# Expert programs of one engine: a fixed place for the second half of each program's code, and one branch hint fewer

## The reference

```python
logits = x @ w_gate
expert_idx = np.argmax(logits, axis=1)
...
h = np.maximum(np.einsum('ecd,edf->ecf', disp, w1), 0.0)
y = np.einsum('ecf,efd->ecd', h, w2)
...
out[i] = gate_w[i] * y[expert_idx[i], pos[i]]
```

## Time and profile before

| what | value |
|---|---|
| median of 3 runs | 406.74 us (404.05 to 407.35) |
| time of the profiled execution | 404.03 us |
| its span, first to last instruction | 402.3 us |
| PE busy | 390.4 us, 97% |
| granted clock of TensorE | 0.999 |
| experts, from the first program's jump to the end | from about 266 to 402 us |

### The profile page before, as it was taken

How to read it: one execution, slowest core, us unless ns; L and a number is a source line. 1 busy time by engine, 2 the same in 40 slices (tenths; PEclk the granted TensorE clock), 3 DMA queues, 4 the chain that set the end, 5 groups by cost and what they waited for, 6 DMA issues and landing times.

```text
span 402.3 us, 7811 instructions
## 1 busy us (share of the span) xinstructions
PE 390.4 (97%) x2876; PEld 372.0 (92%) x2876; DVE 247.9 (62%) x546; ACT 212.4 (53%) x453; POOL 181.5 (45%) x172
## 2 busy tenths in 40 slices
PE   8999999999999999999999999989999999899996
PEld 4999989899999999999999999578999998899995
DVE  5976766745457755457755664658764475786422
ACT  3727766437435236435243333239865577886432
POOL 3865514510304030201039900264896578987542
PEclk9999999999999999999999999999999999999999
DMA  8999968221504051000046140177778787685010
GB/s 216 371 359 338 370 195 297 51 99 51 152 0 150 2 149 51 0 2 2 0 119 219 40 119 2 65 173 232 200 230 224 205 241 240 212 265 148 0 52 21
DMA packets 22716, 58.96 MB, mean 147 GB/s; under 512 B 3332, under 2 KB 8134, under 8 KB 22412
## 3 DMA queue, kind: packets, MB, share of 16 engines
q1 hardware_dynamic: 19052, 50.99, 40.7%
q0 software_dynamic: 2304, 5.77, 5.4%
q10 hardware_dynamic: 1312, 1.52, 1.1%
HBM read 52.46 MB, written 7.91 MB: 150 GB/s over the span
## 4 chain that ended last, share of the span: by engine, by line
PE 91%; DVE 3%; DMA 2%; issue 1%; ACT 1%; POOL 1%; POOLq 0%; SPq 0%; ACTq 0%
PE bank L1410 22%; PE bank L1418 11%; PE bank L1392 10%; PE bank L1393 9%; PE bank L1394 9%; PE bank L1297 5%; PE bank L1396 5%; PE bank L1395 5%; PE bank L1250 3%; PE bank L1280 2%; PE bank L1338 2%; PE bank L1266 2%; PE bank L1535 2%; DMA w2r<-in_w 1%; DMA xg<-xd,idg 1%
## 5 line engine op out<-in xcount | busy, mean ns | idle before, releaser
L798 ACT ACTIVATE tt<-bank 128x384 f32<-128x384 f32 x64 | 31.3, 489 | 76.7 <-PE bank L1396 74.6
L1135 DVE TENSOR_TENSOR g<-bank,tt 128x384 f32<-128x384 f32 x64 | 35.6, 557 | 46.6 <-ACT tt L798 46.3
L1151 DVE TENSOR_TENSOR gl<-g,gh 128x384 fp32r<-128x384 f32 x64 | 41.7, 652 | 29.1 <-ACT gh L808 29.0
L1410 PE MATMUL bank<-woh,gh 128*128 128x328 f32 (+1 forms) x189 | 59.1, 322 | 0.2 <-ACT gh L808 0.2
L1410 PE MATMUL bank<-wol,gh 128*128 128x328 f32 (+1 forms) x189 | 57.2, 311 | 0.0
L1167 DVE SCALAR_TENSOR_TENSOR gl<-bank,gh 128x384 fp32r<-128x384 f32 x64 | 35.4, 555 | 32.2 <-ACT gh L827 31.9
L560 POOL TENSOR_TENSOR w2l<-w2r,w2h 128x640 fp32r<-128x640 f32 x28 | 44.1, 1576 | 23.8 <-DVE w1l L896 23.5
L808 ACT ACTIVATE gh<-g 128x384 fp32r<-128x384 f32 x64 | 33.5, 523 | 37.0 <-DVE g L1135 37.0
L827 ACT ACTIVATE gh<-bank 128x384 fp32r<-128x384 f32 x64 | 31.4, 491 | 30.0 <-PE bank L1396 29.2
L551 POOL TENSOR_TENSOR y<-hs,eo 128x320 f32<-128x320 f32 x11 | 9.0, 815 | 82.1 <-DVE hs L961 71.2
L1392 PE MATMUL bank<-xh,wih 128*128 128x384 f32 x124 | 44.3, 357 | 0.0
(11 more groups left out here) (239 smaller groups left out, 1000.8 us busy)
## 6 DMA issues: line engine op xcount, KB each, us to landing
w1r<-in_w SPq DMA_DIRECT2D x32, 384.0 KB, 3.7
w2r<-in_w SPq DMA_DIRECT2D x32, 320.0 KB, 4.6
qkt<-in_qk SPq DMA_DIRECT2D x12, 416.0 KB
ee<-gsc SPq DMA_DIRECT2D x9, 512.0 KB, 8.8
nat<-in_nat SPq DMA_DIRECT2D x12, 372.0 KB, 7.9
wir<-in_w_in SPq DMA_DIRECT2D x4, 768.0 KB, 12.8
wt<-in_w_out_turned SPq DMA_DIRECT2D x2, 1536.0 KB, 15.9
wor<-in_w_out SPq DMA_DIRECT2D x4, 656.0 KB, 14.1
```

Source lines behind the costliest of these rows:

```text
L1135: ve.tensor_tensor(g[m % 2][:], ps_h[m % 2][:, 0:TM], tt[m % 2][:], ALU.max).then_inc(s_g, 1)
L1151: ve.tensor_tensor(gl[m % 3][:], g[m % 2][:], gh[m % 3][:].bitcast(F32), ALU.subtract)\
L1410: last = mm(parts[s], gh[m % 3][:, cols], w[:, f, 0:parts[s].shape[1]], start=f == 0 and i == 0, stop=False, skip_group_check=True)
```

## The change

```diff
+            BLOCK_AT = {1: (6, 86), 2: (FE, 108), 3: (FE, 88)}
...
             def arm(e, nt, nt_next):
-                near = pe.mark_branch_hint_location()
...
-                return near
...
                             if f == 4 and e + 1 < E:
                                 hints = announce(held[e + 1])
+                            if f == BLOCK_AT[nt][0] and e + 1 < E:
+                                pe.addr_align(256, offset=BLOCK_AT[nt][1], max_nops=0)
                             h_step(M2 + e * FE + f, nt)
...
                         if e + 1 < E:
+                            if FE == BLOCK_AT[nt][0]:
+                                pe.addr_align(256, offset=BLOCK_AT[nt][1], max_nops=0)
                             with pe.If_lt(held[e + 1], one):
-                                near = arm(e, nt, 1)
-                                pe.br(program(e + 1, 1)).branch_hint(hints[0]).branch_hint(near)
+                                arm(e, nt, 1)
+                                pe.br(program(e + 1, 1)).branch_hint(hints[0])
```

More of the change, by code:

```diff
@@ L1767, in _ @@
                         if e + 1 < E:
+                            if FE == BLOCK_AT[nt][0]:
+                                pe.addr_align(256, offset=BLOCK_AT[nt][1], max_nops=0)
                             with pe.If_lt(held[e + 1], one):
-                                near = arm(e, nt, 1)
-                                pe.br(program(e + 1, 1)).branch_hint(hints[0]).branch_hint(near)
+                                arm(e, nt, 1)
+                                pe.br(program(e + 1, 1)).branch_hint(hints[0])
                             with pe.Else():
                                 with pe.If_lt(held[e + 1], few):
-                                    near = arm(e, nt, 2)
-                                    pe.br(program(e + 1, 2)).branch_hint(hints[1]).branch_hint(near)
+                                    arm(e, nt, 2)
+                                    pe.br(program(e + 1, 2)).branch_hint(hints[1])
                                 with pe.Else():
-                                    near = arm(e, nt, 3)
-                                    pe.br(program(e + 1, 3)).branch_hint(hints[2]).branch_hint(near)
+                                    arm(e, nt, 3)
+                                    pe.br(program(e + 1, 3)).branch_hint(hints[2])
                         else:
```

## The result

The changed kernel takes 407.04 us, the median of 16 runs (405.59 to 413.34). The kernel before, run beside it, takes 404.29 us, also the median of 16 (402.82 to 408.98). The ratio is 1.0067 with a 95% interval of 1.0042 to 1.0093: about 2.7 us slower, where 2.2 us faster were forecast. The profiled execution of the changed kernel took 407.11 us.

What follows compares the result with a forecast made beforehand. PE's own work bounds the kernel (busy 97% of the span). -2.8 (experts 3, 4) + 0.3 (expert 5) + 0.3 (padding branches) = -2.2 us, from the 406.74 us median to 404.5 us; range 401.0 to 408.5.

Steps and rivals of the forecast that it cites:

- Gain, two misses: Far branches ending experts 3 and 4 (3.25 and 3.07 us) would find their target fetched in time: 2.80 us gained.
- Experts 0, 1, 2 and 6 lose nothing visible on PE now, so there is nothing to gain there: Far branches ending these four experts: no PE time lost before the change, so no gain counted, 0 us.
- its target's packet cannot be asked for sooner than now: Expert 5's jump from nt 1 to nt 3 stays late: 0.63 us loss remains and grows by 0.3 us (0 to 0.7).
- The branches over the padding: One added branch in each of seven programs, mostly covered by PE's queue: +0.3 us, between 0 and 1.1.
- What is next late: With PE 3 us earlier, the weight pieces on DVE and POOL come next but are not met: no cost.
- Median: The whole kernel's median was 2.7 us above the profiled execution; this unexplained difference was carried over, giving 404.5 us.
- Rival (a): Longer runs before had one or two more far-branch misses; a fixed layout recovers those too: 401.8 us, chance 0.20.
- (b): At the far branches the near hint, not the far hint, brought the target; five more miss: +6.7 us, 413.4 us, chance 0.12.
- (c): Fetch starts late behind the new block's entry; expert 3 stays missed, expert 4 at best late: 406 to 407.3 us, chance 0.15.

Runs made afterwards that it cites:

- mix: Changed kernel with new slots for nt 1 programs alone (40, for expert 6 61), so only their arms lie in one block: 407.43 us, ratio 1.0001.
- arms-in-block kernel: Changed kernel with slots 40, 50, 14 (expert 6: 61, 71, 14), all arms and far branches in the entered block: 405.60 us, ratio 0.9929; again 0.9956.

## Why the prediction was wrong

**Gain, two misses: right.** Forecast 1.25 + 1.55 us; the stages of experts 3 and 4 fell by 1.21 and 1.52, on branches of 0.66 and 0.39 us.

**"Experts 0, 1, 2 and 6 lose nothing visible on PE now, so there is nothing to gain there": this step failed.** I read it as "nothing changes" and put 0 for expert 1, which lost 2.50 us. I had the fact before me: the branch to `nt` 3 lies 40 to 67 slots into "the block behind it". I counted that only for the far branch's target. The block behind is itself code, and it too has to be brought in: its packet began at 294.3 us, and PE stood for 1.49 us. In a program with `nt` 2, as expert 1's, it is needed right after the entry, because the comparisons jump over the arms for `nt` 1 and 2 and land 14 slots ahead of it. Four runs carry this: the arms moved into one block bring expert 1 back to 16.38 and, again, to 16.42 us; the entry moved two steps earlier with the border left where it was, to 16.35; the mix leaves it at 18.91.

**Expert 5, "its target's packet cannot be asked for sooner than now", +0.3 us (0 to 0.7): the same failure.** Measured +2.32 us. That this step's direction was right helps little: I priced the 14 slots by how long the sequencer takes to issue them, 0.7 us, and not by how long it waits for blocks. Its entry lies two steps ahead of the arms, so the stop at the border held PE up by only 0.15 us, but the target's packet came at 364.1 us, 2.1 us behind that stop, where it came at 361.4 before. The quoted sentence holds for this layout alone: with the arms in one block the branch took 0.40 us. How large the loss is differs from one profile to another: stage 5 took 16.35, 15.58 (near hints kept) and 15.01 us (run again), against 14.03 before. Together the two experts cost 4.8 us where 0.3 was set down, and that alone turns the forecast of -2.2 into about +2.3.

**The branches over the padding, +0.3 us (0 to 1.1): close to 0.** They took 0.20 to 0.39 us each on the sequencer, more than the 0.2 assumed:

```profile
L1761 PEldq COMPARE_BRANCH  x3: 317/333/389, 275.7 to 357.1; - x3
L1772 PEldq COMPARE_BRANCH  x4: 201/262/322, 291.7 to 381.2; - x4
```

PE's queue covered them all: stages 0, 2, 4, 6 and 7 show no new cost, and no gap stands behind them at step 6. The feared place was one border too early. The last sentence of the prediction had a stall at the padding branch "if the block that it enters had not been fetched"; that block was there, and the one behind it was not. With these 0 us the sum is +2.1 us, as the stages say.

**What is next late: partly wrong.** It was DVE's xeh at expert 5 (PE waited 0.31 us), seen once the branch there took 0.40 us.

**Median: the carry-over failed by itself.** The 2.7 us between the profiled execution and the median of three was scatter: over 16 runs the kernel before has 404.29 us, 0.3 above the profiled one. With the sum alone, -2.2 on 404.3, I would have forecast 402.1. That the measured 407.04 us lies inside the stated 401.0 to 408.5 is luck, two errors that went against each other. Rival (a) rested on that same scatter and fell.

**Rivals (b) and (c).** (b) fell with the far hint alone (0.9992). That the far hints bring their targets is shown for the six long jumps, which take 0.39 to 0.47 us with hints (arms in one block) and 3.3 to 3.9 us without. It is not shown for the seventh, expert 6's: its target is in the next block in sequence, and it takes 0.30 us with a hint and 0.29 without. So the 0.33 us branch of the earlier trace rows, which is this one, says nothing for the hints; the 0.41 us branch does. (c) gave 406 to 407.3 us and its number was hit by luck: it counted from 406.74 us, a change of -0.7 to +0.6, and +2.7 was measured. Its course was missed too: it wanted expert 3 still missed, and expert 3 was cured. Its mechanism, a fetch that starts late behind an entry, is real at another place. In the changed kernel the first instruction packet lies 1.6 to 3.2 us behind the entry at experts 0, 1, 3, 4 and 5, and in the arms-in-block kernel 0.8 to 1.9 us at all seven. The longest, 3.2 us, is expert 0's, which lost nothing; at experts 1 and 5 it is 2.3 and 2.1 us. What decides there is not an unusually late packet but a second block that is needed behind the first.

## What to carry to other kernels

Where code is laid out by hand, count every block that the sequencer enters between the hint and the jump's target, and not only the block of the target: in these runs each came with a packet of its own, and where a branch or PE waited for it, went on 2.3 to 2.7 us behind the packet's start. Put the comparisons and all arms with their branches into one block that is entered ahead of them (two steps ahead in the `nt` 1 programs here, where one step left a gap of 0.32 us at expert 5); a jump over arms that landed 14 slots short of a border cost most here, 2.50 us. The same goes for the start of a program that is reached by an unannounced jump: five or six slots short of a border, it made PE wait 2.4 to 4.3 us more. And a branch that costs PE nothing today is no proof that its surroundings may be moved: ask what the new layout adds there too.

## What the runs showed that I had not expected

- The near hint shows no effect, within 0.4%: taken out, 0.9992 (0.9956 to 1.0029); kept in the new layout, 1.0056, like the change itself (1.0067).
- An instruction packet was once long in coming. In the kernel with early `nt` 2 entries expert 5's came only at 362.46 us, 4.5 to 5.5 us after the border was crossed between 357.0 and 358.0 us (by the count of slots). From 359 to 361 us the other two queues have 48.7 and 22.1% of the DMA engines' time, from 362 to 364 us 71.6 and 5.5%. That the packet queues behind theirs is only argued; no run took that load away.
- Behind some standstills of PE the granted clock was lower: 1.91 us and then a stage 1.5 us longer (above). In the kernel with early `nt` 2 entries 2.85 us, then a granted clock of 0.88 and 0.69 in the windows 362 to 366 and 366 to 370 us and a stage 6 of 23.13 us instead of 21.58. Behind the 1.76 us of the changed kernel's first profile it stayed at 1.00, and so it did behind 2.05 and 1.98 us in that layout without hints. What decides isn't shown.
- With a start just ahead of a border a missing hint was much dearer. Such programs stopped a second time, for 2.4 to 4.3 us, and the kernel is 39.5 us slower (445.8 against 406.3 for the one before), where the layout with starts far from a border is 12 us slower than before (418.74 against 406.71). Of the 39.5 us, 28.8 are PE's waits at the jumps and borders (20.4 + 7.5 + 0.9). Most of the rest is the clock, which was 0.50 behind five of the six second stops: the granted clock is 0.965 in this profile, 0.987 to 1.000 in most runs of the kernel before on that chip, some 13 us by an estimate from these (0.03 of 444 us).
